# Attention worked two units at a time: order of the TensorE stream, buffers and the routing steps between

## What is computed

```python
scores = scale * np.matmul(q, k.transpose(0, 1, 3, 2))
pos = np.arange(S)
is_sink = pos[None, :] < int(n_sink)
rel = pos[:, None] - pos[None, :]
in_window = (rel >= 0) & (rel < int(window))
scores = np.where(is_sink | in_window, scores, -1000000000.0)
scores = scores - np.max(scores, axis=-1, keepdims=True)
a = np.exp(scores)
a = a / (np.sum(a, axis=-1, keepdims=True) + 1e-09)
return np.matmul(a, v).astype(np.float32)
```

## Time and profile before

| | us |
|---|---|
| median of 3 runs (977.02 to 978.31) | 977.6 |
| the profiled execution | 978.24 |
| its span, first to last instruction | 976.6 |
| of it: start, to the transposes of unit 4 | 21.4 |
| attention's steady part, 90 units | 196.4 |
| last `values` to `up_first` | 3.8 |
| the rest, from `up_first` at 226.32 to the end | 750.3 |

### The profile page before, as it was taken

The page is one execution under the profiler, slowest core; times in us unless marked ns, Lnnn a source line. Parts: engine busy times, 40 slices in busy tenths (PEclk is TensorE's granted clock), DMA queues, the critical chain, the costliest instruction groups (busy, mean ns, idle before and its releaser), DMA issues.

```text
span 976.6 us, 15554 instructions
## 1 busy us (share of the span) xinstructions
PE 945.5 (97%) x5140; PEld 747.8 (77%) x5140; DVE 402.3 (41%) x1302; ACT 313.4 (32%) x759; POOL 95.6 (10%) x175
## 2 busy tenths in 40 slices
PE   6999999999999999999999779999999999999998
PEld 3676777765588888888888568888888888888886
DVE  5777686876522223522223663213123123032120
ACT  4666767663411113311113441211211212112111
POOL 3112222133000000000000140100100100000000
PEclk9999999999999999999999989999999999999999
DMA  4445655375611111611111040200200200100001
GB/s 134 145 166 168 205 174 198 105 232 189 235 55 43 43 43 43 215 43 43 43 43 43 32 119 1 65 22 1 75 11 0 86 0 1 43 1 22 22 0 46
DMA packets 32868, 77.00 MB, mean 79 GB/s; under 512 B 4400, under 2 KB 6448, under 8 KB 32816
## 3 DMA queue, kind: packets, MB, share of 16 engines
q1 hardware_dynamic: 21440, 48.50, 14.8%
q0 software_dynamic: 6080, 19.93, 6.5%
q10 hardware_dynamic: 5296, 7.92, 2.2%
HBM read 52.74 MB, written 23.59 MB: 78 GB/s over the span
## 4 chain that ended last, share of the span: by engine, by line
PE 72%; DMA 1%; POOL 0%; issue 0%; DVE 0%; ACT 0%; ACTq 0%; POOLq 0%
PE bank L586 22%; PE bank L588 22%; PE bank L587 22%; PE bank L615 2%; PE bank L697 1%; PE bank L581 1%; POOL yr L490 0%; DMA yr<-y_sorted,pos_out 0%; DMA y_sorted<-y 0%; DVE yT_lo L1463 0%; DVE y L1386 0%; DVE xT_lo L1368 0%; ACT yT_hi L991 0%; ACT o_sb L1012 0%; DVE yr L1456 0%
## 5 line engine op out<-in xcount | busy, mean ns | idle before, releaser
L588 PE MATMUL bank<-yT_hi,m_lo 128*128 128x512 f32 x432 | 168.1, 389 | 0.0
L827 ACT ACTIVATE probs<-masked,row_min 128x264 f32<-128x264 f32 (+1 forms) x192 | 93.4, 487 | 69.5 <-DVE row_min L1095 66.5
L586 PE MATMUL bank<-yT_hi,m_hi_b 128*128 128x512 f32 x288 | 112.0, 389 | 0.0
L587 PE MATMUL bank<-yT_lo,m_hi_b 128*128 128x512 f32 x288 | 112.0, 389 | 0.0
L1484 DVE TENSOR_TENSOR b_sb<-bank,a_sb 128x512 f32<-128x512 f32 x36 | 24.9, 692 | 187.7 <-PE bank L588 187.7
L588 PEld LDWEIGHTS bank<-yT_hi,m_lo 128*128 128x128 f32 x432 | 81.1, 188 | 16.8
L997 ACT ACTIVATE gT_hi<-g_sb 128x512 fp32r<-128x512 f32 x36 | 22.7, 632 | 200.1 <-DVE g_sb L1487 200.1
L1095 DVE CUSTOM_DVE_ANT_0 masked<-bank,masks 128x264 f32<-128x264 f32 (+1 forms) x192 | 70.6, 405 | 27.6 <-PE bank L512 26.7
L586 PE MATMUL bank<-w_hi,xT_hi 128*128 128x512 f32 x192 | 76.1, 396 | 1.4 <-DVE xT_lo L1368 1.1
L586 PE MATMUL bank<-w_hi,hT_hi 128*128 128x512 f32 x192 | 76.0, 396 | 0.0
L588 PE MATMUL bank<-w_hi,hT_lo 128*128 128x512 f32 x192 | 74.9, 390 | 0.0
(11 more groups left out here) (207 smaller groups left out, 1540.3 us busy)
## 6 DMA issues: line engine op xcount, KB each, us to landing
w_sb<-in_moe_w SPq DMA_DIRECT2D x6, 2048.0 KB, 9.7
xr<-x_sorted POOLq DMA_DIRECT2D x28, 256.0 KB, 3.0
y_sorted<-y ACTq DMA_DIRECT2D x26, 256.0 KB, 2.0
kT<-in_k_t SPq DMA_DIRECT2D x16, 400.0 KB, 3.7
qT<-in_q_t SPq DMA_DIRECT2D x16, 384.0 KB, 3.0
v_in<-in_v_p SPq DMA_DIRECT2D x16, 384.0 KB, 3.0
out<-o_sb SPq DMA_DIRECT2D x24, 256.0 KB, 2.0
m_sb<-in_moe_w SPq DMA_DIRECT2D x6, 768.0 KB
```

What stands on the lines that cost most here:

```text
L586: pe.matmul(psum, a_hi, b_hi, start=first, stop=False)
L587: pe.matmul(psum, a_hi, b_lo, start=False, stop=False)
L588: return pe.matmul(psum, a_lo, b_hi, start=False, stop=last)
L827: last = act.activation(probs[n % 2][:, hd, 0:win_of(t)], masked[n % 2][:, hd, 0:win_of(t)], ACT.Exp, bias=row_min[:, n % 2, hd:hd + 1], s ...
```

## The change

Every loop of attention runs over 48 pairs of neighbouring units, `k`, with the units 2k and 2k+1 (the blocks 0 and 1, 2 and 3, or 4 and 5 of one pair of heads). PE's iteration keeps its order, with each step done for both units before the next: `turn_probs(k + 1)`, `to_row(k - 1)`, `sinks(k)`, `scores(k + 3)`, `values(k)`. Bank 6 holds both units side by side and is emptied by one copy of 256 columns; bank 5 holds both results of `to_row` and is read by one pair of operations. `probs`, `pT`, `sinkT` and `sink_cols` have four buffers in place of two; `masked` and `row_min` keep two, so `mask` now waits for the `exps` of the unit two before it, and `scores` waits for the masks of the pair before it. The transposes wait for the copies of the pair before. `to_row` comes one pair behind, where it came two units behind. `add_up` runs once a pair. The routing steps of a batch are redistributed over 12 pairs, always behind the pair's copy; `choose_gate` now stands straight before `place_read`, and the star is named in pair 8 of the last batch's 12, where it was before unit 13 of 24. At the start, the masks and scores of units 2 and 3 come behind the branch.

```diff
+    NB = NUNITS // 2
+    BPP = QT // 2
+    BPB = UPB // 2
...
+            def scores(k):
+                if k >= 2:
+                    pe.wait_ge(masked_ready, 4 * (k - 1) + 4)
+                for n in (2 * k, 2 * k + 1):
+                    g, t = divmod(n, QT)
+                    if t == 0:
+                        pe.wait_ge(qk_loaded[g % 2], 32 * (g // 2) + 32)
...
+            def turn_probs(k):
+                if k:
+                    pe.wait_ge(pT_kept, 2 * k)
+                for n in (2 * k, 2 * k + 1):
+                    t = n % QT
...
+            def to_row(k):
+                pe.wait_ge(oT_kept, 2 * k + 2)
+
+                pe.wait_ge(rows_kept, 2 * k + 1)
+                for u in range(2):
+                    pe.matmul(bank[5][:, u * PW:(u + 1) * PW], oT[:, u * P:(u + 1) * P], to_rows[:, k // BPP % PPB, :],
+                              start=True, stop=True).then_inc(rows_ready, 1)
+
...
+            def sinks(k):
+
+                if k:
+                    pe.wait_ge(oT_kept, 2 * k)
+                for n in (2 * k, 2 * k + 1):
+                    g, t = divmod(n, QT)
+                    if t == 0:
...
+            def values(k):
+                pe.wait_ge(pT_kept, 2 * k + 2)
...
+                            if w == hd == n % 2 == 0 and (k == 0 or k % BPP == BPP - 1):
+
+                                mm.then_inc(qk_free, 1)
+                    mm.then_inc(values_done, 1)
...
             with pe.If(near > 0):
+                pe.wait_ge(masked_ready, 4)
+                scores(1)
                 turn_probs(0)
                 scores(2)
                 pe.wait_ge(gate_w_loaded, 32)
                 pe.wait_ge(consts_made, 1)
-                for n in range(NUNITS):
-                    if n + 1 < NUNITS:
-                        turn_probs(n + 1)
-                    b, c = divmod(n, UPB)
-                    if b and c == 10:
+                for k in range(NB):
+                    b, c = divmod(k, BPB)
+                    if k + 1 < NB:
+                        turn_probs(k + 1)
+                    if b and c == RANK + 1:
                         pe.wait_ge(ranks_read, b)
-                    if n >= 2:
-                        to_row(n - 2)
-                    sinks(n)
-                    if n + 3 < NUNITS:
-                        scores(n + 3)
-                    if b and c == 9:
-
-                        pe.wait_ge(rows_kept, n)
+                    if k:
+                        to_row(k - 1)
+                    sinks(k)
+                    if k + 3 < NB:
+                        scores(k + 3)
+                    if b and c == RANK:
+
+                        pe.wait_ge(rows_kept, 2 * k + 1)
                         ranks(b - 1)
-                    values(n)
-                to_row(NUNITS - 2)
-                to_row(NUNITS - 1)
+                    values(k)
+                to_row(NB - 1)
...
+            def exps(k):
+                for n in (2 * k, 2 * k + 1):
+                    t = n % QT
+                    act.wait_ge(masked_ready, 2 * n + 2)
+                    if k >= 2:
+
+                        act.wait_ge(probs_turned, n - 3)
+                        if (n - 4) % QT >= 2:
+                            act.wait_ge(sinks_turned, sinks_until(n - 4) + 1)
+                    for hd in range(2):
+                        last = act.activation(probs[n % 4][:, hd, 0:win_of(t)], masked[n % 2][:, hd, 0:win_of(t)], ACT.Exp,
+                                              bias=row_min[:, n % 2, hd:hd + 1], scale=-1.0,
+                                              accum_out=row_sum[:, t, hd:hd + 1])
+                    last.then_inc(exp_done, 1)
...
+            def keep_pT(k):
+                for n in (2 * k, 2 * k + 1):
+                    width = 2 * P * len(key_tiles(n % QT))
+                    act.wait_ge(probs_turned, n + 1)
+                    act.activation(pT[n % 4][:, 0:width], bank[(4, 7)[n % 2]][:, 0:width], ACT.Copy).then_inc(pT_kept, 1)
...
+            def mask(k):
+
+                for n in (2 * k, 2 * k + 1):
+                    t = n % QT
+                    if k:
+                        dve.wait_ge(exp_done, n - 1)
...
+            def keep_rows(k):
+
+                t, hp, xbuf = 2 * k % QT, k // BPP % PPB, k // BPB % 2
+                both = bank[5][:, 0:2 * PW].rearrange("p (u w) -> p u w", u=2)
+                dve.wait_ge(rows_ready, 2 * k + 2)
...
+            def batch(k):
+                if k == 0:
+                    add_up(0)
+                if k + 1 < NB:
+                    turn_sinks(k + 1)
+                    add_up(k + 1)
+                if k:
+                    keep_rows(k - 1)
+                if k + 3 < NB:
+                    mask(k + 3)
+
+                dve.wait_ge(values_done, 2 * k + 2)
+                dve.tensor_copy(oT[:, :], bank[6][:, 0:2 * P]).then_inc(oT_kept, 2)
 
...
                     choose_first(b)
-                elif c == 3:
                     choose_onehot(b)
-                elif c < 7:
-                    count_before(b, range(2 * (c - 4), 2 * (c - 4) + 2))
-                elif c == 7:
+                elif c < 5:
...
+                    batch(k)
+                    if k == 2:
+                        modality_bias()
+                    if b and c < RANK:
+                        route(b - 1, c)
+                    if b and c == RANK:
+                        route(b - 1, c)
+                        place_read(b - 1)
+                    if b and c == RANK + 1:
                         place_write(b - 1)
-                    if b == B - 1 and c == 11:
+                    if b == B - 1 and c == STAR:
                         star_most()
-                    if b == B - 1 and c == 12:
+                    if b == B - 1 and c == STAR + 1:
                         star_index()
-                    if b == B - 1 and c == 13:
                         star_flag()
-                    unit(n)
-                    if b and c == 9:
-                        place_read(b - 1)
-                    if n == 4:
-                        modality_bias()
-                    if b and 1 <= c < 9:
-                        route(b - 1, c - 1)
-                keep_rows(NUNITS - 2)
-                keep_rows(NUNITS - 1)
+                keep_rows(NB - 1)
                 choose(B - 1)
                 place(B - 1)
```

More of the change, by code:

```diff
@@ L399, in _ @@
                           ).then_inc(windows_made, 1)
-            for i in range(2):
+            for i in range(4):
                 pool.memset(sinkT[i][:, :], 0.0)
@@ L505, in _ @@
         def _(pe):
[L506 to L520, removed]
-                    for w in range(len(key_tiles(t))):
-                        col = (len(key_tiles(t)) * hd + w) * P
-                        at = w * (win_of(t) - P)
-                        mm = pe.transpose(bank[(4, 7)[n % 2]][:, col:col + P], probs[n % 2][:, hd, at:at + P], ident[:, :])
-                mm.then_inc(probs_turned, 1)
-            def to_row(n):
-                pe.wait_ge(oT_kept, n + 1)
-                pe.wait_ge(rows_kept, n + 1)
-                pe.matmul(bank[5][:, 0:PW], oT[n % 2][:, :], to_rows[:, n // QT % PPB, :], start=True, stop=True
-                          ).then_inc(rows_ready, 1)
@@ L534, in sinks @@
[L534 to L540, removed]
-                if t >= 2:
-                    pe.wait_ge(sinks_spread, sinks_until(n) + 1)
-                    pe.matmul(bank[6][:, 0:P], v_sink[g % 2][:, :],
-                              sink_cols[n % 2][:, :, :].rearrange("p a c -> p (a c)"), start=True, stop=False,
-                              skip_group_check=True)
@@ new lines, in values @@
+            def values(k):
+                pe.wait_ge(pT_kept, 2 * k + 2)
+                for n in (2 * k, 2 * k + 1):
+                    g, t = divmod(n, QT)
+                    tiles = key_tiles(t)
+                    for w, tile in enumerate(tiles):
+                        for hd in range(2):
+                            col = (len(tiles) * hd + w) * P
+                            mm = pe.matmul(bank[6][D * hd:D * hd + D, n % 2 * P:n % 2 * P + P], v_in[g % 2][:, tile, D * hd:D * hd + D],
+                                           pT[n % 4][:, col:col + P], start=t == 0 and w == 0, stop=w == len(tiles) - 1,
+                                           skip_group_check=True)
+                            if w == hd == n % 2 == 0 and (k == 0 or k % BPP == BPP - 1):
+                                mm.then_inc(qk_free, 1)
+                    mm.then_inc(values_done, 1)
@@ L562, in ranks @@
             def ranks(b):
                 pe.wait_ge(onehot_ready, b + 1)
-                pe.matmul(bank[5][:, 256:256 + QT * E], before[:, :],
+                pe.matmul(bank[5][:, RANKS:RANKS + QT * E], before[:, :],
                           onehots[:, bass.ds(b, 1), :, :].rearrange("p b t e -> p (b t e)"),
                           start=True, stop=False)
```

(9 more changed lines are left out.)

166 lines of the change are left out of this document (78 added, 88 removed).

## The result

The changed kernel takes **963.3 us** (median of 4 runs, 962.4 to 963.3) against 977.6 before, a ratio of 0.9852 (95% interval 0.9838 to 0.9866): 14.3 us faster, where 22.7 were forecast. It lies 0.3 us above the end of the range. The profiled execution is the fastest of the four, 962.38 us with a span of 960.7; its span is 15.9 us shorter than before, more than the 14.3 of the medians, since the profiled execution before was one above its median.

What follows compares the result with a forecast made beforehand. PE, busy 97% of the span, was taken to bound the kernel. Terms -23.5 + 0.4 + 0.4 + 0 = -22.7 gave 955.5 us against the profiled execution, 954.9 as the median; 8-in-10 range 951.5 to 963.

Steps and rivals of the forecast that it cites:

- Fewer changes of shape: PE in attention: three changes of the array's shape a pair instead of six save 0.50 us in 47 pairs, -23.5 us.
- The second unit's weights are hidden: PE's `scores`: the second unit's first weight load is hidden; if not, 0.11 us a pair returns, 960.1 us, chance 0.08.
- Waits inside attention: PE's waits for the ranks and the copy in attention: +0.3 to +1 us net, 0.4 in the sum.
- the room of 0.15: Copy before `to_row`: ready 0.15 us ahead of need where the transposes are of blocks 0 and 1, otherwise up to 0.37.
- Start: Attention's beginning: longer chain for the first units, pair 1 begins at about 21 us; +0.4 us, bounds -0.5 and +2.
- Handoff: From the last `values` to `up_first`: earlier rows against a later star and its weights; 0 us, bounds -0.7 and +1.
- The clock: At the handoff, a longer pause could keep the clock at half speed for one more stretch: up to 1.7 us more.
- the copy comes late in every pair: Rival: one copy for two units, behind four masks, makes PE wait in attention; 960 to 969 us, chance 0.14.
- a slower ACT: Rival: ACT becomes attention's bound, both copies of a pair standing behind four exponentials; 992 us, chance 0.04.

Runs made afterwards that it cites:

- e3: The changed kernel with PE's sinks, scores and values of a pair done unit by unit again, all else as changed: 983.9 us.
- e5: The changed kernel with both units' sinks together but scores and values unit by unit, five changes of shape a pair: 979.5 us.
- e6: e4 with the last pair's sinks moved before the last but one `to_row`, using bank 0, and the modality bias before units 4 and 5's masks: 953.5 us.
- e4: The changed kernel with a batch's routing moved up, positions and scatters by two pairs, the star by one, loads unchanged: 954.3 us.
- e7: e6 with SP's second load of the star's weights held until the star's rows have landed: 953.0 us.

## Why the prediction was wrong, point by point

- **Fewer changes of shape, -23.5 us: right, a little small.** Without waits a group of six units takes 1.59 us less, where 0.50 a pair makes 1.50; for 47 pairs that is some 24.9 us (an estimate from one group of each kernel). The mean of all groups is 1.47 less, since it holds the larger waits. e3 and e5 take 22.3 and 16.2 us of attention's gain back.
- **The second unit's weights are hidden: right.** The Trainium skill's rule ("TensorE: Matmul & The Clock Gate", packing small matmuls) that a weight load overlaps with a matmul in flight only in another row group does not hold here: `scores` of two units take 1.10 us, four rounds of 0.22 with one load (0.11) and one pause (0.10), in the same two halves of the rows.
- **Waits inside attention, +0.4: too small.** The ranks were right (2.1 against 1.9). What I had missed is a wait of 0.7 us behind pair 2: the modality bias keeps DVE from 29.6 to 31.4, only then do its steps of pair 3 begin, and that pair's copy starts at 33.6, when its `to_row` already waits. In e6, where the bias stands at the start, this wait is gone, but pair 1 begins 0.4 us later (21.5). The last two `to_row` wait 0.6 each, since no transposes hide the copy there; and where the transposes are those of blocks 0 and 1, the room of 0.15 was not quite there (in pairs of that kind `to_row` takes 0.55 until `sinks`, not 0.50). Attention's end moved by 21.9 us where the terms for it, with the start, made 22.7. By the estimate above, waits, start and end together took about 3.0 us, not 0.8; the traces name the ranks (1.3 more than before), the bias (0.7) and the last but one `to_row` (0.6), and the rest is small or open.
- **Start, +0.4: right.** Pair 1 begins at 21.11; 21 was expected.
- **Handoff, 0 with bounds -0.7 and +1: the step that failed.** It measured 6.1. I followed two things to the end, POOL's last `spread_sinks` and the star with its weights, and took the rows' load to hang on the first, so that `xr` would land earlier. The star was earlier than I feared (10.8 us before the last `values` ended, not 6), since it stands behind the copy of pair 43 and not 44. But POOL's load of the rows also waits for all scatters of batch 2, and for these I set up no timetable: the positions are written 15.7 us before attention's end instead of 27.6, six scatters follow at 1.3 us each and more, and SP's 2 MB are issued between them. The load went out 0.7 us behind the last `values`, and beside more weights took 7.4 us, not 3.0. The margin had been 8 us (landed at 213.7, wanted at 221.9), so the profile before showed no wait, and I took a dependency without a wait for one that did not matter. The shorter attention is the smaller part of it: e3, with attention as long as before, already has 4.6 of the 6.1 us (8.5 against 3.8).
- **The clock.** I had allowed 1.7 us for one more stretch at the lower level. It came (6.8 us in place of 3.4), but part of it lay in PE's pause; only the transposes of the rows were longer by 0.6 within the handoff, and the time from `up_first` on was unchanged. The stretch at the handoff before is the 3.4 us from 226.4, too short to lower a figure of the earlier trace rows; the dip there, which I had pointed to, is the one before the third layer.

The rival that the copy comes late in every pair did not come true (7 waits, not forty), nor did a slower ACT. That the number lies where that rival stood is chance; it got there for another reason.

## What to carry to other kernels

Order matmuls so that those in the same shape of the array (whole, halves of its rows, halves of its columns) follow each other: each change cost 0.15 to 0.2 us here, in records that all looked busy, and is read only from start to start. When a stage is shortened or its steps get new places, list every event that the next stage waits for, also those that had landed long before, and redo the clock of each against the new end. Here the new place of one small step, four units later, took 10.4 us of margin, and the faster pace 1.5. Two large loads that wait for the same event collide: hold the one that is needed later.

## What the runs showed of the hardware that was not expected

- Six scatters of 256 KB by POOL, issued 1.3 us apart, had landed under 3 us after the last issue with no weights loading beside them, and 8 us after it when SP's 2 MB load was issued between them. Two 256 KB loads beside another 2 MB load took 7.4 us instead of 3.0.
- In e4, e6 and e7 the stretch at the lower clock that had followed attention did not appear, while the one before the third layer was 17.1, 20.5 and 17.1 us long, 13.7 in the kernels before and after. The one does not stand in for the other: e5 had 6.8 us behind attention and 20.5 before the third layer. The cause was not looked into.
